# A softmax denominator by a two-column sum instead of an add of a constant, and an embedding step moved ahead of the bias

## What is computed

```
scores = scale * q @ k.T ; scores += bias ; scores = where(keep, scores, -1e9)
scores -= max(scores) ; a = exp(scores)
a = a / (sum(a) + 1e-09)
x = a @ v                                   # 2 batches, 8 heads, 768 positions, 64 wide
xn = x / (norm(x) + 1e-6)
en = expert_emb / (norm(expert_emb) + 1e-6)
logits = xn @ en.T / tau ; expert_idx = argmax(logits)
out[mask] = gate_w[mask] * (relu(x[mask] @ w1[e]) @ w2[e])      # 8 experts, 512 -> 1024 -> 512
out2 += p[:, e] * (relu(out @ w1b[e]) @ w2b[e])                 # 4 experts, all rows
```

## Time and profile before

| | |
|---|---|
| median of 3 runs | 923.72 us (922.93 to 924.23) |
| profiled execution: span from first to last instruction | 920.3 us |
| what lies around the span (median less span) | 3.4 us |
| PE busy | 864.0 us (94%) |
| DVE busy | 317.8 us (35%) |
| ACT busy | 219.6 us (24%) |
| POOL busy | 288.0 us (31%) |
| mean granted clock of PE | 0.983 |

### The profile page before, as it was taken

How to read it: one execution, slowest core, us unless ns; L and a number is a source line. 1 busy time by engine, 2 the same in 40 slices (tenths; PEclk the granted TensorE clock), 3 DMA queues, 4 the chain that set the end, 5 groups by cost and what they waited for, 6 DMA issues and landing times.

```text
span 920.3 us, 12898 instructions
## 1 busy us (share of the span) xinstructions
PE 864.0 (94%) x4433; PEld 697.1 (76%) x4434; DVE 317.8 (35%) x775; ACT 219.6 (24%) x476; POOL 288.0 (31%) x162
## 2 busy tenths in 40 slices
PE   7898862899999999899999999999999999999998
PEld 5566542688887788788888888888888888888886
DVE  7888772344434434122221212121212121212212
ACT  3777580013333333212101111111111111111110
POOL 5363415027778877550000370000740000500000
PEclk9999995999999999999999999999999999999999
DMA  6799643126667766540000140000220000001001
GB/s 243 226 310 308 201 137 138 35 70 210 207 197 228 227 193 194 176 146 1 1 0 0 42 142 0 0 0 0 92 91 1 0 0 0 1 0 46 19 26 46
DMA packets 33075, 90.96 MB, mean 99 GB/s; under 512 B 4232, under 2 KB 4616, under 8 KB 33040
## 3 DMA queue, kind: packets, MB, share of 16 engines
q1 hardware_dynamic: 23056, 54.86, 17.9%
q10 hardware_dynamic: 8064, 29.36, 10.1%
q0 software_dynamic: 1920, 6.29, 2.1%
HBM read 72.67 MB, written 17.83 MB: 98 GB/s over the span
## 4 chain that ended last, share of the span: by engine, by line
PE 81%; DMA 6%; DVE 5%; issue 4%; POOL 1%; ACT 1%; SPq 1%; DVEq 0%; ACTq 0%
PE ps L1207 28%; PE ps L1194 28%; PE ps L1151 10%; PE ps L1133 7%; DMA xg<-x_sorted 3%; PE ps L1018 2%; DMA win<-qkv 1%; PE ps L1006 1%; POOL x_sorted L472 1%; PE ps L1032 1%; PE ps L1141 1%; PE ps L1123 1%; ACT arena L527 1%; PE ps L977 1%; DVE den L722 1%
## 5 line engine op out<-in xcount | busy, mean ns | idle before, releaser
L1207 PE MATMUL ps<-ring,h 128*128 128x512 f32 x1152 | 275.9, 390 | 0.0
L1194 PE MATMUL ps<-ring 128*128 (+1 forms) x864 | 256.4, 389 | 0.0
L277 POOL TENSOR_TENSOR ring<-raw,ring 128x1024 fp32r<-128x1024 f32 x96 | 227.7, 2396 | 83.7 <-ACT ring L272 80.8
L1207 PEld LDWEIGHTS ps<-ring,h 128*128 128x128 f32 x1152 | 215.7, 188 | 44.6
L945 DVE SCALAR_TENSOR_TENSOR h<-ps,h 128x512 fp32r<-128x512 f32 x96 | 66.3, 691 | 366.3 <-ACT h L596 366.3
L1194 PEld LDWEIGHTS ps<-ring 128*128 128x128 f32 x864 | 162.0, 188 | 33.8 <-DVE x2b L938 0.2
L596 ACT ACTIVATE h<-ps 128x512 fp32r<-128x512 f32 x96 | 57.6, 600 | 427.3 <-PE ps L1194 427.3
L272 POOL CAST ring<-raw 128x1024 fp32r<-128x1024 f32 x36 | 37.5, 1043 | 381.5 <-PE ps L1194 321.2
L1194 PE MATMUL ps<-x2b,ring 128*128 (+1 forms) x288 | 112.1, 389 | 0.0
L272 ACT CAST ring<-raw 128x1024 fp32r<-128x1024 f32 x60 | 62.2, 1052 | 176.1 <-PE ps L1151 116.2
L1133 PE MATMUL ps<-ring,xT 128*128 x384 | 91.5, 394 | 0.8 <-DVE xT L898 0.6
(11 more groups left out here) (115 smaller groups left out, 528.4 us busy)
## 6 DMA issues: line engine op xcount, KB each, us to landing
raw<-wts ACTq DMA_DIRECT2D x56, 512.0 KB, 4.2
raw<-wts SPq DMA_DIRECT2D x40, 512.0 KB, 3.8
win<-qkv SPq DMA_DIRECT2D x32, 320.0 KB, 4.3
x_sorted<-ring SPq DMA_DIRECT2D x20, 256.0 KB, 5.0
xg<-x_sorted SPq DMA_DIRECT2D x17, 256.0 KB, 3.4
y_sorted<-yrow SPq DMA_DIRECT2D x16, 256.0 KB, 3.9
win<-qkv SPq DMA_DIRECT2D x8, 384.0 KB, 6.1
result<-xrow SPq DMA_DIRECT2D x12, 256.0 KB, 2.1
```

The source lines that it names most:

```text
L277: nc.gpsimd.tensor_tensor(w_part(u, 1)[:, q * CW:q * CW + CW], raw[:, q, :], w_part(u, 0)[:, q * CW:q * CW + CW].bitcast(F32), ALU.subtrac ...
L1194: ins = nc.tensor.matmul(ps[:, 4 + f % 2, :], w_part(u1, wp)[:, k * F + f * P:k * F + f * P + P], x2T(xp, k)[:, bass.ds(g * 512, 512)], st ...
L1207: ins = nc.tensor.matmul(ps[:, t, :], h2[:, f % 2, hp_, t * P:t * P + P], w_part(u1 + 1, wp)[:, f * DM:f * DM + DM], start=(f == 0 and n = ...
```

## The change

The buffer of row sums gets a second column per head. It is filled once with 1e-9; ACT writes its sums into the first column. The denominators are then a sum over the two columns, 128x4 elements to 128x2, in place of an addition of a constant, 128x2 to 128x2. `scale_embeddings` leaves the pipeline's step 1 and stands before mask and bias, for both paths of the program.

```diff
-        sums = sb("sums", [P, DUO, 2])
+        sums = sb("sums", [P, DUO, 2, 2])
...
-                                                   accum_out=sums[:, i, hh:hh + 1])
+                                                   accum_out=sums[:, i, hh, 0:1])
...
+            nc.vector.memset(sums[:, :, :, 1], 1e-9)
+
+            def scale_embeddings():
+                dve.wait_ge(emb_root, 1)
+                step(nc.vector.tensor_scalar(norm_e[:, 2:3], norm_e[:, 1:2], 1e-6, None, ALU.add))
+                step(nc.vector.reciprocal(norm_e[:, 3:4], norm_e[:, 2:3]))
+                nc.vector.tensor_scalar(embn_t, emb_t, norm_e[:, 3:4], None, ALU.mult).then_inc(emb_scaled, 1)
+                nc.vector.memset(lg[:, :, :, :], 0.0)
+                step(nc.vector.memset(turner[:, :, P:], 0.0))
+
+            scale_embeddings()
             dve.wait_ge(const_ready, 16)
...
-                    nc.vector.tensor_scalar(den[:, i % 2, :], sums[:, i, :], 1e-9, None, ALU.add).then_inc(denom_ready, 1)
+                    nc.vector.tensor_reduce(den[:, i % 2, :], sums[:, i, :, :], AX.X, ALU.add).then_inc(denom_ready, 1)
...
-                         {1: scale_embeddings, 3: keep_embeddings, 6: expert_weights}, {squares: 5})
+                         {3: keep_embeddings, 6: expert_weights}, {squares: 5})
             with dve.Else():
                 done[0] = before_paths
-                scale_embeddings()
```

More of the change, by code:

```diff
@@ L639, in _ @@
             dve.wait_ge(bias_built, 1)
[L641 to L647, removed]
             def keep_embeddings(idle_times=2):
```

## The result

The changed kernel takes **928.65 us**, the median of 10 runs (926.04 to 934.37); the kernel before, in turn with it, 923.49 (10 runs, 917.59 to 926.50). The ratio is 1.0070, 95% interval 1.0051 to 1.0089: slower by 0.7%, where 912.5 us was forecast. The time lies outside the range of 907.0 to 918.5.

The account below looks back on a forecast made before the run. PE was taken to bound the kernel, held up in attention by denominators waiting for POOL. Gains of 3.8 + 4.3 + 0 + 3.1 = 11.2 us took the median of 923.7 to 912.5 us, range 907.0 to 918.5.

Parts of the forecast that it names:

- After attention.: Routing, scatter and experts, behind attention: they start earlier as a whole, with nothing gained or lost there.
- tile 1 to 7: Early attention: of 5.2 us excess, 3.8 us gained (1.5 to 5.2), 1.4 lost to a cast and copy waiting for POOL.
- tile 12 to 36: Middle of attention: of 8.1 us excess, 4.3 us gained (0 to 8.1), limited by transfers at 331 GB/s.
- tile 36 to 38: Attention after a window wait: the clock drop costing 1.5 us stays, gain 0 (-1.5 to +1.5).
- tile 38 to 44: Late attention: of 4.6 us excess, 3.1 us gained (0 to 4.6), after charges for squares and bias scaling.
- The reduction itself.: Denominators on DVE: the reduction costs between -0.02 and +0.03 us a tile against an undisturbed addition; taken as 0.
- The third rival: Attention's denominators: the reduction waits for POOL as well, gain under 1 us, 923.2 us; chance 0.07.
- The moved embeddings.: Start of the kernel: the scaling fits in DVE's wait for the constants, about 0.6 us of cover left, cost nothing.
- the slower rival: Tile 12 to 36: transfers drop to 281 GB/s, windows starve PE and its clock falls, 926.4 us; chance 0.03.
- the one for the squares: Tile 38 to 44: 0.9 us charged because the first squares (L680) come while POOL still works.
- the one for the bias scaling: Tile 38 to 44: 0.6 us charged because the last head pair's bias scaling (L710) comes while POOL still works.

Follow-up runs that it names:

- Run 2: The kernel before with only 96 unused bytes added behind `nmax`, no edit of attention: 942.44 us, ratio 1.0204.
- run 5: The changed kernel with the wider `sums` last in attention's memory and 96 unused bytes in its old place, all else at old addresses: 911.11 us, ratio 0.9893.
- run 3: The kernel before with only the denominator by reduction, plus 32 bytes of padding (total shift 128): 924.59 us, ratio 1.0006.
- run 4: The kernel before with only the embeddings' scaling moved ahead of mask and bias, at the old addresses: 925.64 us, ratio 1.0002.
- Run 1: The changed kernel with 32 more unused bytes behind `nmax` (total shift 128): 926.81 us, ratio 1.0019.
- run 9: The kernel before with 96 unused bytes in front of `ring`, so weights and operands move together: 927.44 us in one execution.
- run 8: The kernel before with 96 unused bytes in front of `h2` alone: 927.67 us in one execution.

## Why the prediction was wrong

**The step that failed** is the part "*After attention.*", with its last sentence, "Nothing gained or lost". It counted instructions, and there is none in that part that the change touches. What it left out is that a wider `sums` moves the tiles that the experts' products read: 16.8 us in the profiles. Run 2 (the shift without the edits) and run 5 (the edits without the shift) show it, and price it at 17.8 and 16.4 us in medians (942.44 less 924.65; the change's 5.2 lost and run 5's 11.3 gained). No rival had it. The last sentence of the prediction names "if the experts' part gets longer" as what would prove it wrong, but no chance and no price stood behind it. The result is the sum of two: 6.8 us less up to the first expert product and 16.8 more behind it, which makes the 10.0 us between the spans.

**The rest of the sum** can be read in run 5, where the products are as before. Its scores, PE's timeline of run 5 (tiles 1, 7, 12, 36, 38, 44, 47):

```profile
11.54 0.70 PE L1008 MATMUL ps<-win 64*128 64x256 f32 x4
...
26.02 0.70 PE L1008 MATMUL ps<-win 64*128 64x256 f32 x4
...
37.91 0.70 PE L1008 MATMUL ps<-win 64*128 64x256 f32 x4 [1.18 <-DMA win<-qkv]
...
91.22 0.70 PE L1008 MATMUL ps<-win 64*128 64x256 f32 x4 [0.17 <-DMA win<-qkv]
...
95.33 0.70 PE L1008 MATMUL ps<-win 64*128 64x256 f32 x4
...
107.69 0.70 PE L1008 MATMUL ps<-win 64*128 64x256 f32 x4
...
115.37 0.70 PE L1008 MATMUL ps<-win 64*128 64x256 f32 x4
```

| stretch | forecast gain | run 5 | changed kernel |
|---|---|---|---|
| tile 1 to 7 | 3.8 | 3.0 | 3.1 |
| tile 7 to 12 | 0 | -0.8 | -1.9 |
| tile 12 to 36 | 4.3 | 4.2 | -0.1 |
| tile 36 to 38 | 0 | 1.5 | 1.5 |
| tile 38 to 44 | 3.1 | 4.6 | 4.6 |
| tile 44 to 47 | not counted | -1.5 | -1.1 |
| tile 1 itself | 0 | 0.1 | -0.3 |
| sum | 11.2 | 11.1 | 5.8 |

*The reduction itself.* Right: 0.157 us against the 0.170 assumed, under POOL or not. The Trainium skill, "SBUF — State Buffer", section "Who interferes with whom", has it that a `tensor_reduce` on this chip never contends. The trace agrees: 48 of 48 took at most 0.16 us in each of the seven traces that have it. The Trainium skill's rule against `tensor_reduce` on a hot path ("VectorE: DVE Perf Modes", "Rules for kernel authors") would have decided wrongly here: at four elements the reduction took 0.157 us where the addition took up to 2.29. The third rival, a reduction that waits, is out.

*The moved embeddings.* Right on the cost: ready at about 5.3. In the changed kernel 1.01 us of cover was left, since the constants came at 6.34, and in run 5, where they came at 6.00, just the 0.60 that was worked out. But they bring nothing measurable by themselves (runs 3 and 4): tile 1 to 7 has 1.7 us of excess in run 3, without the move, and 6.2 in run 4, with the move alone. The forecast had given them a part of the 5.2 us.

*Tile 1 to 7.* Right in mechanism, 0.8 too high. The cast ended with POOL's subtraction, as foretold, and the copy behind it waited as well, which was not priced.

*Tile 12 to 36.* In run 5 as forecast, 53.3 us for 53.2, at the rate of this row of its stretches:

```profile
40.00:98.00 58.00, 54.81 (x473) 37.04 (x472) 42.50 (x241) 48.06 (x161) 24.72 (x16) 1.00 0.94 323
```

323 GB/s at 0.94 busy, for 331 and 0.96. In the changed kernel's trace nothing is gained, since two waits of 2.24 and 1.95 us came before tiles 12 and 17, and the step behind each took 3.6 us in place of 2.06. That is the slower rival's mechanism, in a weaker form and at other tiles (it had 18, 24 and 30): the rate was 294 GB/s, not 281. It cost that profile some 4 us, and isn't what made the kernel slower; at the old addresses the same instructions gain the 4.2. Run 1 had 5.4 us of excess there and run 3 6.6, so the size differs from run to run, and what decides whether a window comes late stays open.

*Tile 38 to 44.* Of the two charges, the one for the squares was right in kind and too early in place, and the one for the bias scaling was wrong. DVE and POOL side by side in run 5:

```profile
106.29 2.01 DVE L683 CUSTOM_DVE_ANT_0 win<-xrow 128x512 f32<-128x512 f32 x1
...
109.09 0.69 DVE L713 TENSOR_SCALAR arena<-arena 128x1024 f32<-128x1024 f32 x1
```

```profile
105.39 2.35 POOL L278 TENSOR_TENSOR ring<-raw,ring 128x1024 fp32r<-128x1024 f32 x1
107.69 1.50 POOL L273 CAST ring<-raw 128x1024 fp32r<-128x1024 f32 x1
109.27 2.74 POOL L278 TENSOR_TENSOR ring<-raw,ring 128x1024 fp32r<-128x1024 f32 x1
```

A square, 0.68 us alone, takes 2.01 under the subtraction; the step that it delays is that of tile 44 (3.38 us), so the 1.5 us stand behind the stretch and not in it. POOL's cast, issued while the square was in work, took 1.50 for 1.04. The bias scaling never waited: L712 took 693 to 694 ns all four times in the changed kernel. Here it was first, at 109.09, and the subtraction behind it took 2.74 for 2.35. The 0.6 us charged for it were wrong.

*The sum.* Run 5 saved 11.3 us (922.38 less 911.11) where 11.2 was forecast, closer than the parts deserve: tile 36 to 44 gave 3.0 more than forecast, the other stretches 3.1 less.

## What to carry to other kernels

Before a buffer is widened, or one is added, look at what is allocated behind it: every tile there moves, also one that belongs to a later part of the program. Where an edit is judged, compare the duration of instructions that it did not touch first; here a few ns on each of 3,072 products hid a real gain of 11 us, and allocating the widened buffer last gave it back. Keep the tiles that PE reads together at the same place within 256 bytes, as here, or measure what another one costs.

## What the runs showed that I had not expected

- **PE's pace depends on where its two operands start against each other.** At a granted clock of 1.00, products of `h` with `ring` start every 226.7 ns when `h2` is shifted by 0 or 256 bytes, 233.2 at 32, 234.5 at 96, 231.9 at 128; 226.6 when it is moved by 96 and the weights with it (run 9). Up to 3.4%. Other distances (64, 160, 192, 224) were not tried. Why it costs is not shown. Products with both operands in `ring` slow by less (226.4 to 230.1, and to 228.4 when only `h2` is moved); in run 8 the slow ones are those just behind a product of `h`.
- **Two inputs in SBUF are enough to wait for POOL.** The square of a tile with itself went from 0.68 us to 1.68 in the changed kernel and 2.01 in run 5. Here is the row of the changed kernel by source line, shortest, median and longest in ns:

```profile
L682 DVE CUSTOM_DVE_ANT_0 win<-xrow x6: 683/688/1683, 112.0 to 129.0; 128x512 f32<-128x512 f32 x6
```

  The Trainium skill, "SBUF — State Buffer", section "Who interferes with whom", says so of two inputs in SBUF beside a GpSimd operation that reads SBUF. These rows agree; no row before the change had shown it.
- **The clock fell in the midst of attention.** PE stood still for 2.24 and for 1.95 us, and behind each the granted clock was 0.50 (1.2 GHz) and one step took 1.5 us more. In run 5, with waits of 1.18 and 1.36 us, it stayed at 1.00 from 0 to 98.
